# A long-convolution kernel: the filter network's 64 hidden channels are transformed, and W2 is applied to their spectrum

## What is computed

```python
h_mlp = np.maximum(pos_emb @ w1, 0.0) @ w2          # (S,64) -> (S,64) -> (S,128)
window = np.exp(-0.01 * pos)[:, None]
h_filt = h_mlp * window
u = x * v
Uf = np.fft.rfft(u, n=2*S, axis=1)
Hf = np.fft.rfft(h_filt, n=2*S, axis=0)
y = np.fft.irfft(Uf * Hf[None, :, :], n=2*S, axis=1)[:, :S, :]
x = x * y
x = (np.maximum(x @ w_in, 0) ** 2) @ w_out           # moe
h = x @ w_in2; out = (h * sigmoid(1.702 * h)) @ w_out2   # moe2
```

## Time and profile before

| | us |
|---|---|
| median of 3 runs | 1452.71 |
| lowest and highest run | 1450.67, 1452.84 |
| the profiled execution's own time | 1449.64 |
| its span, first to last instruction | 1447.9 |
| TensorE busy | 1432.8 |
| ScalarE busy | 1018.6 |
| VectorE busy | 877.9 |
| GpSimd busy | 190.7 |

### The profile page before, as it was taken

The page is one execution under the profiler, slowest core; times in us unless marked ns, Lnnn a source line. Parts: engine busy times, 40 slices in busy tenths (PEclk is TensorE's granted clock), DMA queues, the critical chain, the costliest instruction groups (busy, mean ns, idle before and its releaser), DMA issues.

```text
span 1447.9 us, 22467 instructions
## 1 busy us (share of the span) xinstructions
PE 1432.8 (99%) x7980; PEld 1395.2 (96%) x7980; DVE 877.9 (61%) x1119; ACT 1018.6 (70%) x1453; POOL 190.7 (13%) x143
## 2 busy tenths in 40 slices
PE   8999999999999999999999999999999999999998
PEld 6998999899999999999999999999999999999997
DVE  3667526764666666666666666666666666666664
ACT  6665346545777777777777777777777777777775
POOL 5517630715000000000000000000000000000000
PEclk9999999999999999999999999999999999999999
DMA  7314850545000000000000000000000000000000
GB/s 213 97 35 116 208 144 15 151 142 154 1 18 19 18 18 18 18 18 18 18 18 18 18 18 18 18 18 18 18 18 18 18 18 18 18 18 18 6 7 12
DMA packets 35016, 63.73 MB, mean 44 GB/s; under 512 B 4228, under 2 KB 27252, under 8 KB 34724
## 3 DMA queue, kind: packets, MB, share of 16 engines
q1 hardware_dynamic: 34440, 62.69, 15.2%
q10 hardware_dynamic: 540, 0.55, 0.1%
HBM read 50.45 MB, written 6.39 MB: 39 GB/s over the span
## 4 chain that ended last, share of the span: by engine, by line
PE 97%; DVE 1%; ACT 1%; issue 0%; DMA 0%; SPq 0%; ACTq 0%
PE ps L1053 25%; PE ps L1054 25%; PE ps L1055 25%; PE ps L768 6%; PE ps L813 6%; PE ps L778 4%; PE ps L397 4%; PE ps L749 2%; PE ps L742 1%; DVE act_lo L1041 0%; PE ps L734 0%; PE ps L756 0%; ACT act_f L994 0%; ACT act_hi L997 0%; DMA big<-in_pos_emb 0%
## 5 line engine op out<-in xcount | busy, mean ns | idle before, releaser
L1041 DVE TENSOR_TENSOR act_lo<-act_f,act_hi 128x832 fp32r<-128x832 f32 x480 | 489.7, 1030 | 124.5 <-ACT act_hi L997 116.2
L1053 PE MATMUL ps<-in_hi,w_hi 128*128 128x416 f32 x960 | 338.3, 352 | 4.1 <-DVE big L405 1.7
L1053 PE MATMUL ps<-act_hi,w_hi 128*128 128x416 f32 x960 | 338.5, 353 | 0.7 <-DVE act_lo L1041 0.7
L1055 PE MATMUL ps<-act_hi,w_lo 128*128 128x416 f32 x960 | 336.5, 351 | 0.0
L1054 PE MATMUL ps<-act_lo,w_hi 128*128 128x416 f32 x960 | 336.5, 351 | 0.0
L1054 PE MATMUL ps<-in_lo,w_hi 128*128 128x416 f32 x960 | 336.2, 350 | 0.0
L1055 PE MATMUL ps<-in_hi,w_lo 128*128 128x416 f32 x960 | 334.6, 349 | 0.0
L1039 DVE CAST act_hi<-act_f 128x832 fp32r<-128x832 f32 x240 | 144.4, 602 | 295.3 <-ACT act_f L992 295.3
L987 ACT ACTIVATE relu<-ps 128x832 f32<-128x832 f32 x240 | 208.3, 868 | 133.2 <-PE ps L1055 129.6
L994 ACT ACTIVATE act_f<-ps 128x832 f32<-128x832 f32 x240 | 207.1, 863 | 105.0 <-PE ps L1055 104.9
L992 ACT ACTIVATE act_f<-relu 128x832 f32<-128x832 f32 x240 | 216.2, 901 | 24.1 <-DVE act_lo L1041 2.1
(11 more groups left out here) (66 smaller groups left out, 1057.9 us busy)
## 6 DMA issues: line engine op xcount, KB each, us to landing
f_ring<-in_fwd SPq DMA_DIRECT2D x52, 240.0 KB, 2.6
big<-in_inv SPq DMA_DIRECT2D x23, 338.0 KB
big<-in_x_by_channel SPq DMA_DIRECT2D x16, 390.0 KB
big<-in_v_by_channel SPq DMA_DIRECT2D x16, 390.0 KB
x_tile<-in_x_by_tile SPq DMA_DIRECT2D x30, 208.0 KB, 2.7
xy_tile<-big SPq DMA_DIRECT2D x60, 104.0 KB, 2.5
out<-yT SPq DMA_DIRECT2D x30, 208.0 KB, 1.9
big<-in_pos_emb SPq DMA_DIRECT2D x40, 78.0 KB
```

The source lines that it names most:

```text
L1041: nc.vector.tensor_tensor(lo[:, :, :], f[:, :, :], hi[:, :, :].bitcast(F32), ALU.subtract)\
L1053: nc.tensor.matmul(to, w_hi[w][:, cols], hi, start=first, stop=False)
L1055: return nc.tensor.matmul(to, w_lo[w][:, cols], hi, start=False, stop=last)
```

## The change

The filter network's last product is linear, so it may follow the transform. The front now ends at the 64 hidden channels after the relu; these are transformed once, and W2 is applied to their spectrum for each half.

- `pos_emb` arrives from the host laid out by row pairs, with the 128 (row of the pair, channel) on the partitions (`by_pair`). The transposes and the copy after them are gone. The front has 15 rounds of four pairs, and a round is four products with W1 of 128 columns (`hidden_layer`, L730), four relus of the high rows on ScalarE with the ratio of the decays as scale (`relu_high`, L591), and two fused relu-and-fold operations on VectorE (L677, L678). The decay of the low row is applied in step 1's copies.
- `H` has 64 channels for both halves. Step 1 has 16 groups of filter and 16 of input in the first half, and 16 of input in the second (`N1`). Its wait for u is now for the piece at hand, and for three pieces at first (L744).
- Step 2 of the first half makes the hidden spectrum (`hidden_spectrum`, L787), which ScalarE copies to `HID` (L625), then the input's spectrum (L797) and the W2 product on `HID` (L803), four products each per group. The hidden spectra use slots 0 and 2 and the products slots 1 and 3. In the second half only L797 and L803 remain, in all four slots. The loops over groups are written out.
- GpSimd clears the four zero columns of each piece of u by itself (L546).
- The memory plan is new. With it SyncE's order changes: all of `pos_emb` goes ahead of u; five pieces of the second half's u are loaded among step 2's tables of the first half; only two of step 4's table groups are loaded ahead of step 3's end instead of five; and the first two weight matrices are loaded in the second half's step 2, ahead of its last two table groups.

```diff
-N1, N3 = 2 * HC // 4, HC // 4
+N1, N3 = (2 * HC // 4, HC // 4), HC // 4
...
-    net = np.concatenate([twice(w1), twice(w2), np.repeat(decay_b, FO, axis=0)], axis=1)
+    net = np.concatenate([twice(w1), np.tile(ratio, (128, 1))], axis=1)
+    out_net = np.concatenate([by_row, -by_row, twice(w2[:, :HC]), twice(w2[:, HC:])], axis=1)
...
+def by_pair(z):
+
+    rows = z.reshape(A, B, FO)
+    return np.stack([rows[:, :LOW], rows[:, :LOW - 1:-1]]).transpose(0, 3, 2, 1).reshape(2 * FO, LOW * A)
...
+    def hidden_slot(k):
+
+        return 2 * (k % 2), used["s2", 0][2 * (k % 2)] + k // 2
+
+    def product_slot(k, h):
+
+        q = k % RING if h else 2 * (k % 2) + 1
+        return q, used["s2", h][q] + (k // RING if h else k // 2)
...
-            sp.dma_start(pe_rows[:, n, 0:HB], pe_d[:, ds(n * HB, HB), :]).then_inc(ld_pe[n], 16)
-            sp.dma_start(pe_rows[:, n, HB:CB], pe_d[:, ds(B - HB - n * HB, HB), :]).then_inc(ld_pe[n], 16)
+            cols = slice(n * PB * A, (n + 1) * PB * A)
+            sp.dma_start(pe_t[:, n * PB:(n + 1) * PB, :].rearrange("p j a -> p (j a)"), pe_pairs[:, cols])\
+                .then_inc(ld_pe[n], 16)
...
+        for n in range(NCH):
+            load_pe(n)
+        for i in range(PIECES):
+            load_u(0, i)
+        for k in range(RING):
+            load_f(0, k)
+        stage_done(sp, "s1", 0)
+        for k in range(RING, NG):
+            load_f(0, k)
+            if k % RING == RING - 1:
+                load_u(1, k // RING - 1)
+
+        p_made(sp, 0)
+        stage_done(sp, "s2", 0)
+        for g in range(2):
+            load_t4(sp, 0, g)
+        sp.dma_start(t4_last[0], inv4[:, JG * TB * TAB:]).then_inc(t4_last_in, 16)
+        sp.dma_start(w2bd, out_net[:, 2 + D:]).then_inc(w2_in, 16)
+
+        stage_done(sp, "s3", 0)
+        for g in range(2, T4S[0]):
+            load_t4(sp, 0, g)
+        sp.wait_ge(u_folded, PIECES + 4 + 1)
+        load_u(1, 5)
+        load_t4_behind(0, range(T4S[0], JG))
+        sp.wait_ge(u_folded, PIECES + 3 + 1)
+        load_u(1, 6)
+        sp.wait_ge(u_folded, PIECES + 5 + 1)
+        load_u(1, 7)
+
+        stage_done(sp, "s4", 0)
+        for k in range(NG - 2):
+            load_f(1, k)
+        for m in range(2):
             load_w(m)
+        for k in range(NG - 2, NG):
+            load_f(1, k)
...
+            nc.gpsimd.memset(to[:, :, LOW:ODD], 0.0)
...
-        def copy_pe(n):
-            s, i = n % RING, n // RING
-            act.wait_ge(pe_trans[s], i + 1)
-
-            after(act, hid_made[s], i)
-            nc.scalar.copy(peT[:, s], slot[s][:, 0, 0:HB * A]).then_inc(pe_copied[s], 1)
-
-        def relu_hid(n):
-            s, i = n % RING, n // RING
-            act.wait_ge(hid_made[s], i + 1)
-
-            after(act, full[s], i)
-            for j in range(HB):
-                cols = slice(j * A, (j + 1) * A)
-                last = nc.scalar.activation(hid[:, s, cols], slot[s][:, 1, cols], ACT.Relu, scale=decay[:, n, j:j + 1])
-            last.then_inc(hid_relu[s], 1)
-
-        def copy_high_rows(n):
+        def relu_high(n):
             s, i = n % RING, n // RING
             act.wait_ge(full[s], i + 1)
 
             after(act, free[s], i)
-            nc.scalar.copy(high_rows[:, s], by_channel(flat[s][0:A, HB * D:CB * D].rearrange("p (b c) -> p b c", b=HB)))\
-                .then_inc(high_copied[s], 1)
+            for j in range(PB):
+                last = nc.scalar.activation(high_rows[:, s, :, j], flat[s][0:A, (2 * j + 1) * FO:(2 * j + 2) * FO],
+                                            ACT.Relu, scale=ratio[0:A, n * PB + j:n * PB + j + 1])
+            last.then_inc(high_made[s], 1)
...
+            def copy_hidden(k):
+                q, n = hidden_slot(k)
+                act.wait_ge(full[q], n + 1)
+                nc.scalar.copy(HID[:, k * FG:(k + 1) * FG, :],
+                               slot[q][:, 0, 0:FG * B].rearrange("p (f b) -> p f b", f=FG)).then_inc(free[q], 1)
...
+                if h == 1 and k >= 2:
+                    before, n = product_slot(k - 2, h)
+                    act.wait_ge(free[before], n + 1)
...
+            low = flat[s][0:A, 0:PB * 2 * FO].rearrange("p (j e o) -> p e o j", j=PB, e=2)[:, 0]
+            high, rows = high_rows[:, s], slice(n * PB, (n + 1) * PB)
+            dve.wait_ge(high_made[s], i + 1)
+            nc.vector.scalar_tensor_tensor(H[:, :, rows], low, 0.0, high, ALU.max, ALU.add)
+            nc.vector.scalar_tensor_tensor(H[:, :, ODD:BR][:, :, rows], low, 0.0, high, ALU.max, ALU.subtract)\
...
-            pe.wait_ge(ld_pe[n], 2 * 16)
+            pe.wait_ge(ld_pe[n], 16)
             after(pe, free[s], i)
-            for j in range(HB):
-                mm = nc.tensor.transpose(slot[s][0:128, 0, j * A:(j + 1) * A],
-                                         pe_rows[:, n, 2 * j:2 * j + 2, :].rearrange("p b c -> p (b c)"),
-                                         ident[0:A, 0:A])
-            mm.then_inc(pe_trans[s], 1)
-
-        def first_layer(n):
-            s, i = n % RING, n // RING
-            pe.wait_ge(pe_copied[s], i + 1)
-            nc.tensor.matmul(slot[s][:, 1, 0:HB * A], w1bd.rearrange("p e n -> p (e n)"), peT[:, s],
-                             start=True, stop=True).then_inc(hid_made[s], 1)
-
-        def second_layer(n):
-            s, i = n % RING, n // RING
-            pe.wait_ge(hid_relu[s], i + 1)
-            for j in range(HB):
-                mm = nc.tensor.matmul(flat[s][0:A, j * 2 * D:(j + 1) * 2 * D], hid[:, s, j * A:(j + 1) * A],
-                                      w2bd.rearrange("p e n -> p (e n)"), start=True, stop=True)
+            for j in range(PB):
+                mm = nc.tensor.matmul(flat[s][0:A, j * 2 * FO:(j + 1) * 2 * FO], pe_t[:, n * PB + j, :], w1bd,
+                                      start=True, stop=True)
...
-            if k == N1 // 2:
-
-                pe.wait_ge(u_folded, (h + 1) * PIECES)
+            q, c = k % RING, 4 * k % HC
+            filtered = of_filter(k, h)
+            if not filtered:
+
+                pe.wait_ge(u_folded, h * PIECES + (c // PC + 1 if h else max(c // PC + 1, 3)))
...
+            def hidden_spectrum(k):
+                s, (q, n) = k % RING, hidden_slot(k)
+                pe.wait_ge(ld_f[s], 16 * (k // RING + 1))
+                pe.wait_ge(free[q], n)
                 for j in range(FG):
-
-                    mm = nc.tensor.matmul(flat[s][0:B, j * 2 * D:(j + 1) * 2 * D], f_ring[0:BR, s, j, :],
-                                          Z[h][:, :, ds((k * FG + j) * 2 * HC, 2 * HC)],
+                    mm = nc.tensor.matmul(slot[q][:, 0, j * B:(j + 1) * B],
+                                          ZH[:, k * FG + j].rearrange("p r o -> p (r o)"), f_ring[0:BR, s, j, :],
                                           start=True, stop=True)
-                mm.then_inc(full[s], 1)
-
-            rounds(pe, NG, step2)
+                mm.then_inc(full[q], 1)
+
+            def step2(k):
+                s, (q, n) = k % RING, product_slot(k, h)
+                pe.wait_ge(ld_f[s], 16 * (h * F_USES[s] + k // RING + 1))
+                pe.wait_ge(free[q], n)
+                for j in range(FG):
+                    nc.tensor.matmul(flat[q][0:B, (2 * j + 1) * D:(2 * j + 2) * D], f_ring[0:BR, s, j, :],
+                                     ZU[:, k * FG + j].rearrange("p r c -> p (r c)"), start=True, stop=True)
+                if h == 0:
+                    hidden, n = hidden_slot(k)
+                    pe.wait_ge(free[hidden], n + 1)
+                for j in range(FG):
+                    mm = nc.tensor.matmul(flat[q][0:B, 2 * j * D:(2 * j + 1) * D], HID[:, k * FG + j, :], w2bd,
+                                          start=True, stop=True)
+                mm.then_inc(full[q], 1)
+
+            if h == 0:
+                hidden_spectrum(0)
+            for k in range(NG):
+                if h == 0 and k + 1 < NG:
+                    hidden_spectrum(k + 1)
+                step2(k)
```

More of the change, by code:

```diff
@@ L218, in mlp_buffers @@
-    skip_to(Y_AT[1] + Y_SIZE)
+    assert at[0] <= Y_AT + (JG - LATE) * TB * 2 * D
+    skip_to(Y_AT + Y_SIZE)
     out["relu"] = put("relu", pair)
     out["yT"] = put("yT", [128, TN])
-    out["act_f"] = [put("act_f0", pair)]
-    assert at[0] <= T4_AT and SPEC_AT[1] + SPEC <= T4_AT
+    assert at[0] <= X_AT[1]
+    skip_to(W_LO2_AT)
+    out["w_lo"][2] = put("w_lo2", [128, DFF], F32R)
+    out["xy_tile"][1] = put("xy_tile1", [128, TN])
+    assert at[0] <= X_AT[0]
+    skip_to(P_AT[1])
+    for m in range(4):
+        out["w_hi"][m] = put(f"w_hi{m}", [128, DFF], F32R)
@@ new lines, in mlp_buffers @@
+    out["w_lo"][3] = put("w_lo3", [128, DFF], F32R)
+    for n in range(2):
+        out["in_hi"][n] = put(f"in_hi{n}", [128, TN], F32R)
+        out["in_lo"][n] = put(f"in_lo{n}", [128, TN], F32R)
+    out["stage"] = put("stage", [128, TN])
+    out["x_tile"][0] = put("x_tile0", [128, TN])
+    out["xy_tile"][0] = put("xy_tile0", [128, TN])
```

(48 more changed lines are left out.)

363 lines of the change are left out of this document (138 added, 225 removed).

## The result

| | before | after |
|---|---|---|
| median of 4 runs, us | 1451.91 | 1426.36 |
| lowest and highest run, us | 1450.67, 1452.84 | 1425.07, 1429.64 |
| the profiled execution's own time, us | 1449.64 | 1425.94 |
| TensorE busy, us | 1432.8 | 1406.5 |

The account below looks back on a forecast made before the run. TensorE, busy 99% of the span, was taken as the bound. The terms -28.8 + 24.1 + 0.5 - 22.6 + 0.6 + 3.0 = -23.2 us gave 1452.71 - 23.2 = 1429.5 us, range 1424 to 1440.

Parts of the forecast that it names:

- The front, -28.8: Products before step 1: 15 rounds of 0.88 us on TensorE, so step 1 starts at 21.4 instead of 50.18 us.
- the rise: Start of the front: TensorE's first products run at half speed until 8 us, by when 2.4 rounds are done.
- The bound of 1.38 us a round: ScalarE's four relus in the front, if they do not overlap; step 1 would then start at 27.4 us.
- u, zero: First half's step 1: GpSimd folds u by 59.6 us, TensorE wants the eighth piece at 63.8; no cost, 4 us cover.
- Step 2, first half, +24.1 and +0.5: 26 groups of 2.66 us make 69.3 us against 45.1, plus 0.5 for late tables, 0 to 5 possible.
- the line: TensorE's pace per record follows its moving columns, 0.00083 us per column, so 128 columns give 0.110 us.
- The 0.113 of step 4: Pace of 32 records of 104 columns, read as a floor set by 128 weight columns and applied to L787.
- Step 4, 0 to 1: First half: the eleventh table is there at 20.2 us, wanted at 20.5 after step 3; zero, at worst 1 us.
- The second half's step 1, -22.6, and step 2, +0.6 and +3.0: 16 groups of step 1 gone; step 2 takes 45.8 us, and its table stalls behind two weight matrices, 2.8 to 3.7 us.
- the table passes the weights: Rival, second half's step 2: the table does not queue behind the weights, the 3.0 us go, 1426.5 us; chance 0.13.
- the clock falls in the stall: Rival, second half's step 2: half speed after the stall costs 2.1 us more, 1431.6 us; chance 0.06.
- Weight loads that stop hiding: Rival, step 2: 624 more loads no longer overlap; a full 0.1 us each gives 1491 us, slower than before; chance 0.04.

Follow-up runs that it names:

- the early load: Changed kernel, with a one-column relu on ScalarE ahead of the first round so its table loads early: 1427.18 us, ratio 0.9845.
- one wait for all: Changed kernel, with TensorE's step 1 waiting for all eight pieces of u instead of the piece at hand: 1450.3 us, ratio 0.9989.
- both orders: Changed kernel, second half's step 2 tables ahead of the weights and first half's step 4 tables ahead of u's sixth piece: 1419.97 us.
- the changed kernel again: The changed kernel run once more with no edit, against the kernel before on the same chip: 1425.28 us, ratio 0.9836.
- another execution: Profiled run of the changed kernel with only one weight matrix ahead of the last two tables, the other behind: 1429.51 us; that kernel's median 1420.67.
- the split product: Kernel before, with each step 2 product cut into two of 128 columns on the same table: 1450.36 us, ratio 1.0002.
- the four edits: Changed kernel, tables ahead of weights, step 4 tables ahead of u's sixth piece, ScalarE's table early, second half's x and v issued apart: 1420.88 us.

## Why the prediction was right, point by point

I set the starts of the stages against each other, so that each difference holds a stage and the products behind it: -28.0 for the front, 71.60 - 47.90 = +23.7 for the first half's step 2, +0.6 for its steps 3 and 4, 24.01 - 46.52 = -22.5 for the second half's step 1 and 52.52 - 47.89 = +4.6 for its step 2. Together -21.6 us, which is how much earlier the dense networks start.

- *The front, -28.8.* It came to -28.0 (50.18 to 22.18). TensorE sets it, as the sum has it: it has no wait in its 120 records, and from the fourth round on ScalarE starts as soon as TensorE has filled the slot. The term that was mis-sized is the rise: the fast pace was put at 8 us and came at about 10, so that TensorE is through at 20.3 and not at 19.1. Behind it stand 1.9 us and not 2.3. In the ten profiled executions with this front (two of them with the early load) the fast pace came between 7 and 10 us and step 1 started between 20.89 and 22.18, so a single profile says little here to a microsecond. The bound of 1.38 us a round was far off: the first eight relus take 1.81 us, about 0.2 apart, so a round is 0.8 us of ScalarE against 0.88 of TensorE.
- *u, zero.* Nobody waited. GpSimd's timeline has a new piece every 4.67 us, and the last folded at 53.45 + 1.20 = 54.65 us instead of 59.6, because the first piece had landed at 17 us and not at 22:

```profile
17.07 0.12 POOL L546 MEMSET big<- 104x32 f32 x1 [16.02 <-DMA big<-in_v_by_channel]
...
21.84 0.12 POOL L546 MEMSET big<- 104x32 f32 x1
...
26.51 0.12 POOL L546 MEMSET big<- 104x32 f32 x1
...
53.45 1.20 POOL L550 TENSOR_TENSOR big<-big 104x480 f32<-104x480 f32 x1
```

The run with one wait for all showed what hung on the wait by pieces: the whole gain. TensorE wanted the eighth piece at about 64 us, so the cover was some 10 us and not 4.

- *Step 2, first half, +24.1 and +0.5.* +23.7, and no late table in this execution (0.38 us once with both orders). L797 and L803 pace at 0.110 as forecast. L787 does as well, and not at 0.113; with 120 moving columns the line gives 0.103. The 0.113 of step 4 was read from a stretch that begins behind 0.80 us of idle time and holds a slower first record; the next 32 records, from 177.08 to 180.65 us, are 0.112 apart. That fits one floor of some 0.11 us for weights of 128 columns in both places, but no run varied the width alone.
- *Step 4, 0 to 1.* 0.35 us here, 0.80 in the changed kernel again, and 1.38 us in another execution, where a slow stretch of 17 us followed; none in the other profiles. "At worst 1 us" was the weakest sentence of the working: the wait was bounded a little low, and what can follow a wait was left out.
- *The second half's step 1, -22.6, and step 2, +0.6 and +3.0.* Step 1's 128 records take 22.69 us, half of what 256 took before. Step 2 came to +4.6 where +3.6 was said. The stall was 2.09 instead of 3.0, because w_raw1 landed 7.3 us after its issue and not 8.9; the table landed 0.7 us behind it, as forecast. The clock added 1.76 us. That is the second term that was mis-sized: the sum puts nothing for it.
- *The rivals.* That the table passes the weights is out: the wait goes with the bytes ahead of it. That the clock falls in the stall, at 0.06, happened in this execution, nearly at the price named (2.1 said, 1.76 found), and in two of four profiles with this stall; its chance was too small. Weight loads that stop hiding are out by the split product and by the 0.110 us of after itself, and so is the Trainium skill's rule on them (TensorE: Matmul & The Clock Gate, The mechanism) as the prediction reads it. The same page's section Why this matters for your kernels has the clock fall back behind longer idle gaps; the profiles agree behind 4.13, 9.60 and 10.43 us, and show falls behind 1.38, 2.04 and 2.09 us too, though not behind each wait of that length.
- *What nobody forecast.* The profiled execution is 23.7 us shorter, 2.1 more than the start of the dense networks gives. One microsecond of that is a wait in their first tile, of 1.71 us before:

```profile
328.14 0.45 PE L1051 MATMUL ps<-in_hi,w_hi 128*128 128x416 f32 x1 [0.74 <-DVE big L424]
```

  The wait goes with how long VectorE's cast (`act_hi<-act_f`) ahead of it takes: 2.01 us before and 1.02 after; 2.12 with all tables ahead of the weights, where the wait was 1.81 us again, and 0.60 with the four edits, where it was 0.33. Why the same cast takes so different a time wasn't tried. The rest, 1.1 us of some 1100, is no more than runs differ by.

So the sum came within 2.4 us of the medians' difference and 0.5 of the profiles', the median of 1426.36 lies in the range at its lower end (1424 to 1440), and part of that is luck: the later rise of the front's pace (0.8), the clock in the stall (1.8) and step 4 (0.6) cost more than forecast; the shorter stall (0.9), the tables of the first half (0.5), step 2's pace there (0.4) and the dense networks (2.1) gave it back.

## What to carry to other kernels

Where TensorE is at 99%, moving a linear step behind a transform pays by the records it removes, and the first question is who now waits: here a single wait for a whole stage's input would have eaten all 25 us, and waiting by pieces kept them. Large transfers that nobody needs yet belong behind the small ones that the next stage waits for, and the bytes ahead in the queue tell how late these are. Give even a short wait in the middle of dense TensorE work a price of its own and the clock's on top: 1.4 us of idle time have cost 9 in one execution. And compare more than one profile before a microsecond is put down to an edit: the start of step 1 moved by 1.1 us with nothing changed ahead of it.

## What was not expected of the hardware

- The granted clock fell behind idle times of 1.38, 2.04, 2.09, 4.13 and about 10 us, and did not behind 2.20, 2.14, 1.81 and 0.82; some 3.4 us ran at half speed in one case (behind 2.09) and some 17 in another (behind 1.38). What decides isn't settled by these runs.
- ScalarE's first activation brings a table load of 1.28 us, which runs where that instruction stands in the program: behind the waits ahead of it, if it is not brought forward. In this kernel the engine catches up with it, and an estimated 0 to 0.4 us is what the late load costs.
- 416 more weight loads of 120 columns in two stages of 45 us each lengthen each stage by 0.5 us and could not be measured in the kernel's time, within 0.1%.
- In the front of the changed kernel TensorE's records came 0.213 us apart up to a point between 7 and 10 us, another in each profile, and 0.110 from there.
